# A fused recurrence and two mixing layers in fp32: scores asked for one chunk ahead, split units and moved weights

## The reference, cut to what matters

```python
# attention, per batch (4) and head (8), 768 steps, head size 48
state = alpha[t][:, None] * state + k[t][:, None] * v[t][None, :]
y[t] = q[t] @ state
x = y as (4, 768, 384)
# first mixing layer
theta = x @ w_theta
y = w_tok_r @ (x * cos(theta)) + w_tok_i @ (x * sin(theta))
u = x + y
x2 = u + relu(u @ w_ch)
# second mixing layer, d_ff = 1024
h = relu(x2 @ w_in); u, v = h[:, :512], h[:, 512:]
out = (u * (w_spatial @ layernorm(v) + b)) @ w_out
```

## Time and profile before

| what | value |
|---|---|
| median of 3 runs | 590.03 us (589.51 to 591.0) |
| the profiled execution | 590.33 us, span 588.6 us |
| PE busy | 576.1 us, 98% of the span |
| DVE, ACT, POOL busy | 69%, 42%, 38% |
| granted clock of PE | 1.00 throughout |

### The profile page before, as it was taken

How to read it: one execution, slowest core, us unless ns; L and a number is a source line. 1 busy time by engine, 2 the same in 40 slices (tenths; PEclk the granted TensorE clock), 3 DMA queues, 4 the chain that set the end, 5 groups by cost and what they waited for, 6 DMA issues and landing times.

```text
span 588.6 us, 11251 instructions
## 1 busy us (share of the span) xinstructions
PE 576.1 (98%) x4577; PEld 547.6 (93%) x4577; DVE 407.4 (69%) x627; ACT 247.0 (42%) x462; POOL 221.6 (38%) x184
## 2 busy tenths in 40 slices
PE   6899899999999999999999999999999999999998
PEld 5788899999999999999999989998999899989997
DVE  6988998777877877877743279887527762776253
ACT  2767565453544543444434124922431343134210
POOL 2455343342322422422413037374713471347221
PEclk9999999999999999999999999999999999999999
DMA  7952322132322321420233081200220022002002
GB/s 281 325 200 86 118 69 69 40 137 69 108 68 68 109 75 63 167 76 18 92 108 121 1 279 44 81 0 1 82 81 1 0 81 81 0 2 82 0 1 80
DMA packets 21219, 49.53 MB, mean 84 GB/s; under 512 B 1712, under 2 KB 16816, under 8 KB 20656
## 3 DMA queue, kind: packets, MB, share of 16 engines
q1 hardware_dynamic: 21168, 48.81, 24.1%
HBM read 39.37 MB, written 9.44 MB: 83 GB/s over the span
## 4 chain that ended last, share of the span: by engine, by line
PE 89%; DVE 5%; ACT 2%; POOL 1%; issue 1%; DMA 1%; SPq 0%; DVEq 0%; ACTq 0%
PE psY L517 22%; PE psC L549 7%; PE psC L476 5%; PE psY L682 4%; PE psY L633 4%; PE psS L425 4%; PE psY L643 3%; PE psF L459 3%; PE psF L623 3%; PE psS L682 3%; PE psF L682 3%; PE psY L623 2%; PE psF L643 2%; PE psS L643 2%; PE psS L633 2%; PE psF L451 2%
## 5 line engine op out<-in xcount | busy, mean ns | idle before, releaser
L1306 POOL TENSOR_TENSOR z_lo<-cos_sin,z_hi 128x768 fp32r<-128x768 f32 x23 | 43.8, 1902 | 104.7 <-ACT z_hi L796 104.7
L1374 POOL TENSOR_TENSOR gated_lo<-raw_gated,gated_hi 128x384 fp32r<-128x384 f32 x32 | 35.9, 1127 | 71.2 <-ACT gated_hi L927 70.0
L1293 POOL TENSOR_TENSOR akq<-akq 128x512 f32<-128x512 f32 x23 | 27.4, 1193 | 58.8 <-DVE akq L994 58.8
L517 PE MATMUL psY<-tok_r_hi,z_hi 128*128 128x384 f32 x126 | 45.5, 361 | 1.0 <-POOL z_lo L1306 1.0
L1027 DVE SCALAR_TENSOR_TENSOR psC<-turns,psC 128x384 f32<-128x384 f32 x24 | 13.4, 559 | 44.2 <-ACT turns L776 44.2
L1313 POOL TENSOR_TENSOR u_lo<-u_f,u_hi 128x384 fp32r<-128x384 f32 x24 | 23.8, 1019 | 50.1 <-ACT u_hi L801 50.1
L983 DVE TENSOR_TENSOR akq<-akq,after 128x512 f32<-128x512 f32 x24 | 41.8, 1741 | 1.1 <-DMA akq<-akq 0.3
L517 PE MATMUL psY<-tok_i_hi,z_lo 128*128 128x384 f32 x126 | 42.2, 335 | 0.0
L517 PE MATMUL psY<-tok_r_hi,z_lo 128*128 128x384 f32 x126 | 42.2, 335 | 0.0
L517 PE MATMUL psY<-tok_i_hi,z_hi 128*128 128x384 f32 x126 | 42.2, 335 | 0.0
L517 PE MATMUL psY<-tok_i_lo,z_hi 128*128 128x384 f32 x126 | 42.2, 335 | 0.0
(11 more groups left out here) (307 smaller groups left out, 1807.9 us busy)
## 6 DMA issues: line engine op xcount, KB each, us to landing
akq<-akq SPq DMA_DIRECT2D x22, 770.0 KB, 4.4
v<-v_in SPq DMA_DIRECT2D x24, 192.0 KB, 4.6
x_dram<-u_f SPq DMA_DIRECT2D x8, 576.0 KB, 3.7
out<-ot SPq DMA_DIRECT2D x24, 192.0 KB, 1.9
raw_x<-x_dram SPq DMA_DIRECT2D x3, 1152.0 KB, 5.0
raw_tok_r<-w_tok_rT SPq DMA_DIRECT2D x6, 384.0 KB, 7.1
raw_tok_i<-w_tok_iT SPq DMA_DIRECT2D x6, 384.0 KB, 8.7
raw_sp<-w_spT SPq DMA_DIRECT2D x4, 576.0 KB, 6.2
```

What stands on the lines that cost most here:

```text
L517: mm = pe.matmul(psY[:, j, 0:HALF], Z[s][l][:, q, tile(j)], W[m][:, s, half(h)], start=(s == 0 and q == 0 and n == 0), stop=(s == CHUNKS - ...
L1306: pool.tensor_tensor(Z[c][1][:], trigs[g % 2][:], f(Z[c][0][:]), ALU.subtract).then_inc(z_lo, 1)
L1374: pool.tensor_tensor(GA[1][:, j, half(h)], ug[:, j, half(h)], f(GA[0][:, j, half(h)]), ALU.subtract).then_inc(g_lo, 1)
```

## The change

From chunk 12 on (`AHEAD`), PE asks for the scores of chunk g+1 right behind `attend(g)`, and turns its keys right behind `transpose_x(g)`. The load of a chunk's inputs waits for `asked`, set when the queries of the chunk that held the buffer are last read by L451, in place of `attended`. DVE, ACT and POOL have their orders changed to suit: DVE makes the decays of chunk g+2 in chunk g and reduces the angle of g at its end; ACT copies x ahead of `z_high`, and does `u_highs` one slot earlier with `whole_turns` and `sines` behind; POOL likewise. The stores of x2 stand one slot later in SP's order. In chunk 10 DVE and POOL prepare chunk 12 as well as 11. In chunk 6 the first unit is cut into its high parts (12 matmuls, before `keys_values`) and low parts (6, behind `attend`), and the second unit into high parts, then low parts. WN moves from `late_at` to 64 bytes below it.

```diff
-        r = Region(late_at)
+        r = Region(work_at + CHUNKS * G * 4)
         WN = [r("in_hi", [CT, FF], F32R), r("in_lo", [CT, FF], F32R)]
...
-                if g > 2:
+                if g > 4 and (g - 2) % CHUNKS:
+                    sp.wait_ge(asked, (g - 2) // CHUNKS * LINKS + (g - 2) % CHUNKS)
+                elif g > 2:
                     sp.wait_ge(attended, g - 1 if g > 4 else g - 2)
...
-                    if c == 1 and b:
+                    if c == 2 and b:
                         store_x2(b - 1, 1)
-                    if c == 4:
+                    if c == 5:
                         store_x2(b, 0)
...
-                    turn_k(g)
-                    scores(g)
+                    if g < AHEAD:
+                        turn_k(g)
+                        scores(g)
                     if g == CHUNKS:
                         first_mix(ya, range(CT), Z_HIGH)
-                        first_mix(ya, range(CT), Z_LOW)
                     else:
                         token_mix(ya)
                     keys_values(g)
                     attend(g)
+                    if AHEAD <= g + 1 < ALL:
+                        scores(g + 1)
+                    if g == CHUNKS:
+                        first_mix(ya, range(CT), Z_LOW)
                     channel_mix(n, g)
                     transpose_x(g)
+                    if AHEAD <= g + 1 < ALL:
+                        turn_k(g + 1)
...
+                        if g == CHUNKS:
+                            first_mix(yb, range(CT), Z_HIGH)
+                            first_mix(yb, range(CT), Z_LOW)
+                        else:
+                            token_mix(yb)
...
+                    else:
+                        copy_x(g)
+                        z_high(g - 1)
                     xT_high(g)
+                    if AHEAD <= g + 1 < ALL:
+                        copy_kT(g + 1)
...
+                    if g + 1 >= AHEAD:
+                        if c == 0:
+                            u_highs(HALVES * b)
+                        if c == 3:
+                            u_highs(HALVES * b + 1)
+                        whole_turns(g)
+                        sines(g)
...
+                        if g + 2 == AHEAD:
+                            decay_keys(g + 2)
+                            decay_queries(g + 2)
+                        continue
+                    update_state(g)
+                    if g >= AHEAD:
+                        multiply_z(g - 1)
                     if g + 1 < ALL:
-                        decay_keys(g + 1)
-                        decay_queries(g + 1)
+                        mask_scores(g + 1)
                     make_x2(tile_of(b, c))
                     xT_low(g)
-                    update_state(g)
+                    if g + 2 < ALL:
+                        decays_back(g + 2)
                     if c == 0:
                         make_u(HALVES * b)
...
                     if c == 3:
                         make_u(HALVES * b + 1)
+                    if g + 2 < ALL:
+                        scale_keys(g + 2)
+                        decay_queries(g + 2)
+                    reduce_angle(g)
...
-                    if g + 1 < ALL:
+                    if g + 1 < AHEAD:
                         scale_queries(g + 1)
+                    if c == 0 and g >= AHEAD:
+                        u_lows(HALVES * b)
+                    if c == 3 and g >= AHEAD:
+                        u_lows(HALVES * b + 1)
+                    if AHEAD <= g + 2 < ALL:
+                        scale_queries(g + 2)
```

More of the change, by code:

```diff
@@ L55 @@
 PASSES = ((0, 0), (0, 1), (1, 0))
+AHEAD = 2 * CHUNKS
 TOKEN_HALVES = (slice(0, 64), slice(64, P))
@@ L240, in build @@
         k_scaled, q_scaled = sems("k_scaled q_scaled")
-        kT_made, scored, kv_made, attended = sems("kT_made scored kv_made attended")
+        kT_made, scored, kv_made, asked, attended = sems("kT_made scored kv_made asked attended")
         kT_copied, x_copied = sems("kT_copied x_copied")
@@ L450, in attend @@
                         for rows in TOKEN_HALVES:
-                            pe.matmul(psO[rows, pr], Q[akq_of(g)[0]][:, p, rows], S[c % 2][:, p, :],
-                                      start=(p == 0), stop=False, skip_group_check=True)
+                            mm = pe.matmul(psO[rows, pr], Q[akq_of(g)[0]][:, p, rows], S[c % 2][:, p, :],
+                                           start=(p == 0), stop=False, skip_group_check=True)
+                    mm.then_inc(asked, 1)
                 pe.wait_ge(v_arrived[s], 16 * (g // 2 + 1))
@@ L494, in first_mix @@
                             mm = pe.matmul(psY[:, j, 0:HALF], Z[s][l][:, q, tile(j)], W[m][:, s, half(0)],
-                                           start=(s == 0 and q == 0 and n == 0), stop=False)
-                if parts == Z_LOW:
+                                           start=(s == 0 and q == 0 and n == 0),
+                                           stop=(s == CHUNKS - 1 and q == 1 and n == 2))
+                    if parts == Z_LOW and s == CHUNKS - 1:
+                        mm.then_inc(y_made, 1)
+                if parts == Z_LOW and s < CHUNKS - 1:
                     mm.then_inc(mixed, 1)
@@ L605, in _ @@
                     else:
-                        token_mix(yb)
+                        if g == CHUNKS:
[3 more added lines that the diff above has]
+                            token_mix(yb)
                         angles(g, 0 if n is None else n + 1)
@@ L858, in _ @@
                     g = (b + 1) * CHUNKS + c
[L859 to L867, removed]
+                    if g < AHEAD:
+                        whole_turns(g - 1)
+                        copy_kT(g)
+                        if c == 1:
+                            u_highs(HALVES * b)
+                        if c == 4:
+                            u_highs(HALVES * b + 1)
+                        sines(g - 1)
+                        z_high(g - 1)
+                        copy_x(g)
+                    else:
+                        copy_x(g)
+                        z_high(g - 1)
                     xT_high(g)
+                    if AHEAD <= g + 1 < ALL:
+                        copy_kT(g + 1)
                     if g == CHUNKS:
@@ L875, in _ @@
                     spread_state(g)
-            whole_turns(ALL - 1)
-            sines(ALL - 1)
+                    if g + 1 >= AHEAD:
+                        if c == 0:
+                            u_highs(HALVES * b)
+                        if c == 3:
+                            u_highs(HALVES * b + 1)
+                        whole_turns(g)
+                        sines(g)
             act.wait_ge(y_made, HALVES * (BATCH - 1) * CT)
@@ L1106, in _ @@
                     g = (b + 1) * CHUNKS + c
-                    reduce_angle(g - 1)
-                    mask_scores(g)
-                    multiply_z(g - 1)
+                    if g < AHEAD:
+                        reduce_angle(g - 1)
+                        mask_scores(g)
+                        multiply_z(g - 1)
+                        if g + 1 < AHEAD:
+                            decay_keys(g + 1)
+                            decay_queries(g + 1)
+                    if g + 1 < AHEAD:
+                        make_x2(tile_of(b, c))
+                        xT_low(g)
+                        update_state(g)
+                        if c == 0:
+                            make_u(HALVES * b)
+                        if g == CHUNKS + 1:
+                            for i in MID_SPLITS[2:]:
+                                tok_low(i)
+                        if g == CHUNKS:
+                            dve.wait_ge(ch_hi, 1)
+                            dve.tensor_tensor(WC[1][:], raw_ch[:], f(WC[0][:]), ALU.subtract).then_inc(ch_lo, 1)
+                        if c == 3:
+                            make_u(HALVES * b + 1)
+                        if g + 2 == AHEAD:
+                            decay_keys(g + 2)
+                            decay_queries(g + 2)
+                        continue
@@ L1236, in _ @@
             b = BATCH - 1
-            reduce_angle(ALL - 1)
             for n, q in enumerate((1, 0)):
@@ L1339, in _ @@
                     g = (b + 1) * CHUNKS + c
-                    if c == 1:
+                    if c == 1 and g < AHEAD:
                         u_lows(HALVES * b)
-                    if c == 4:
+                    if c == 4 and g < AHEAD:
                         u_lows(HALVES * b + 1)
                     z_low(g - 1)
-                    if g + 1 < ALL:
+                    if g + 1 < AHEAD:
                         scale_queries(g + 1)
+                    if c == 0 and g >= AHEAD:
[4 more added lines that the diff above has]
+                        scale_queries(g + 2)
                     if g == CHUNKS + 2:
```

6 lines of the change are left out of this document (removed).

## The result

| | before | after |
|---|---|---|
| median | 590.29 us (4 runs, 589.51 to 591.0) | 586.05 us (4 runs, 585.54 to 586.9) |
| span of the profiled execution | 588.6 us | 584.7 us |

The ratio is 0.993, with a 95% interval of 0.9911 to 0.9949: faster by 4.2 us by the medians. A second measurement of the changed kernel gave a median of 585.91 us (8 runs, 585.52 to 589.85) and a ratio of 0.9936 (0.9914 to 0.9957).

What follows compares the result with a forecast made beforehand. PE, busy 98% of the span, was taken to bound the kernel. Gains of 0.8 + 1.3 + 1.4 less 0.3 lost make 3.2 us, from 590.33 to 587.1 us profiled, median 586.8, range 585.0 to 588.8.

Steps and rivals of the forecast that it cites:

- both tight places: PE's wait for z_lo in slot 0 (chunks 12 and 18), 0.3 us lost, and DVE's extra decays before chunk 11, cost 0.
- Seventh slot: Chunk 6: low matmuls moved behind `attend` and the second unit split shorten the wait for z_lo; gain 0.8 us.
- Scores behind attention: Chunks 12 to 23: one entry and one exit go, a new L459-to-L425 neighbour costs 0.10; gain 1.3 us.
- Rival 2: Chunks 12 to 23: the new neighbour of small groups is free, another 1.2 us gained, 585.6 us; chance 0.1.
- Weights: L643 and L623: WN moved 64 bytes to a full 128-byte step makes their matmuls faster; gain 1.4 us.
- rival 1: L643 and L623: the weights' place doesn't matter, no 1.4 us gain, 588.2 us; chance 0.25 with its twin.
- its twin: Chunks 12 to 23: merging the scores gains nothing, same time as rival 1, 588.2 us; chance 0.25 together.
- New waits: Slot 0, chunks 12 and 18: PE arrives sooner and waits for z_lo, 0.14 us each; 0.3 us lost.
- Chunk 11: DVE makes chunk 12's decays in chunk 10 too, yet the mask is ready before L459 wants it; cost 0.
- Rival 3: Steady loop: a new wait, as for late scaled queries in slots 1 and 4; 4 us slower, 594 us; chance 0.05.

Runs made afterwards that it cites:

- The experiment before attend: Changed kernel with the next chunk's scores moved from behind `attend` to between `keys_values` and `attend`; 592.13 us in one run.
- the kernel with the split: Changed kernel with the second unit of chunks 12 and 18 also cut into high parts, then low parts; 586.15 us in one run.

## Why the prediction was right, point by point

The forecast was 586.8 us in 585.0 to 588.8, measured 586.05. The sign was right, and so was each term's account of what goes and what comes, with both tight places. Two things behind the numbers were not: the price of coming out of a small group, and the reason why the weights' place matters. The size was 3.2 us where the traces give 4.06; by terms that is 0.71 + 2.5 + 1.24 - 0.4.

- **Seventh slot**: forecast 0.8, measured 0.71. As stated, ACT's queue holds the copy of x, the transposes start as late as before, and the gain is at the second wait. `angles` started 11.36 us into the chunk, 11.38 was forecast. The restart behind that wait took the rest: its nine matmuls took 1.70 us and not 1.56. One thing was missed, a wait of 0.29 us of L464 for the mask; it costs nothing, since PE waits for the copy of x behind it anyway.
- **Scores behind attention**: this term was mis-sized, 1.3 forecast and 0.20 to 0.24 a chunk, about 2.5 us over twelve, measured. The failed step is "it costs 0.10 us to enter a group of half-array matmuls and 0.11 us to come out". I read the 0.11 from the first large matmul behind L459 and took all time before it for the group's own. But the group's last matmul already holds the 0.10 us of a change; coming out costs 0.21. The experiment before attend shows it, where L441 takes 0.60 us before a change and 0.50 without, and so do the single starts: the next group begins 0.15 us behind the last matmul of L459, where the pairs within it follow by 0.05. So L459 paid a change before, towards L549, and L464 pays the same one now, towards L429 (1.02 and 1.01 us). I charged that as new. What went is one change and one restart, 0.20 us a chunk. That a change of shape costs was right, but I had it speak against the gain, though both orders pay it at this place. Rival 2 (a free neighbour) came nearer to the chunk's length, 13.62 us against 13.65, for a wrong reason.
- **Weights**: forecast 1.4, measured 1.24. `gate_inputs` went to 173.3 ns a matmul as said, 0.93 us in all. `values` gave 0.32 and not 0.48: of its 54 matmuls the last 45 take the 226.7 ns of the forecast, but the first nine take 231.2 ns each, and why is open. The reason that I gave, half a step of 128 bytes, fell. By that reason 128 bytes further up would have been as good, and there the last part is 0.7 us longer than in the kernel before, so the choice of this place was luck. That the weights' place matters held, so rival 1 is out, and the 0.20 us a chunk of the moved scores put out its twin.
- **New waits**: forecast 0.3, measured 0.4 (13.86 against 13.65 us, twice). z_lo came 8.35 us after `angles`, as forecast from chunk 18; PE was sooner there than I thought, 8.20 us behind `angles` in the kernel with the split, which doesn't wait there, where I had 8.28.
- **Chunk 11** cost nothing: from L464 of chunk 9 to that of 10 are 13.85 us and from 10 to 11 are 12.93, both as before.
- **Rival 3** had its place right, as the kernel with the scores before attend shows, and didn't come. In the changed kernel the queries are ready at 161.38 + 1.18 = 162.56 us in chunk 13 and wanted at 164.09, 1.5 us of room, where I had counted 0.7. The least room in any of the twelve chunks is 1.3 us. The scaling of keys that the rival took at 2.16 us takes 0.69 to 1.09.

## What to carry to other kernels

When PE is full, look at starts and not at waits: every step between full array and halves, or between two kinds of halves, cost 0.10 us here, and the first large matmul behind halves cost another 0.11. So put small groups side by side, and those of one shape next to each other. Read the price of coming out from both sides of the border, the last matmul of the group included. Where PE passes a tight place sooner, ask which producer is then late; a split into parts that need only the early half of the data takes such a wait away.

## What the runs showed of the hardware that was not expected

- Moving a pair of weight tiles (24 KB in each partition) by 32, 64 or 128 bytes against the other operand changes a stream of 384- or 512-column fp32r matmuls by up to 2.6%, in no order that five places reveal, while moving all tiles together by 64 bytes changes nothing.
- DVE's scaling of keys takes 0.69 us where POOL is idle and 2.16 beside z_lo; POOL in turn took 2.73 us for a split beside DVE's scan and scaling that took it 1.84 just before, and the scan 1.85 in place of 1.23. There the scaling ended 0.55 us behind the end of POOL's split (105.52 and 104.97 us), not far from the 0.69 us that it takes alone. That looks like an instruction that waits for the whole of the other one; no run tests it.
- The price of a change lies at the last matmul before it: 0.15 in place of 0.05 us for L464, 0.20 in place of 0.11 for L429, to the start of what follows.
